# Second attention product of a windowed-attention kernel: 24 products on four 128x32 strips in place of 12 on two 128x64 tiles

## What is computed

```python
# batch 4, heads 8, seq 768, head_dim 64, chunk 32, left 16, right 8, 8 memory keys
for c in range(nc):                        # 24 chunks of 32 queries
    k_full = concat([mem_k, k_ctx])        # 8 + up to 56 = 64 keys
    v_full = concat([mem_v, v_ctx])
    scores = scale * q_c @ k_full.T
    a = softmax(scores)                    # 32 x 64
    out[:, :, c_start:c_end] = a @ v_full  # the second product, 32 x 64 x 64
x = attn_out as (3072, 512)
h = x @ w_in ; solu = h * softmax(h) ; ln = norm(solu) * g ; x2 = ln @ w_out
return leaky(x2 @ w_in2) @ w_out2
```

## Time and profile before

| | us |
|---|---|
| median of 3 runs | 803.44 |
| lowest, highest | 802.81, 803.88 |
| the profiled execution | 801.41 |
| its span, first to last instruction | 799.6 |
| TensorE busy | 792.2 |
| VectorE busy | 541.4 |
| ScalarE busy | 453.8 |

### The profile page before, as it was taken

How to read it: one execution, slowest core, us unless ns; L and a number is a source line. 1 busy time by engine, 2 the same in 40 slices (tenths; PEclk the granted TensorE clock), 3 DMA queues, 4 the chain that set the end, 5 groups by cost and what they waited for, 6 DMA issues and landing times.

```text
span 799.6 us, 14400 instructions
## 1 busy us (share of the span) xinstructions
PE 792.2 (99%) x5582; PEld 650.3 (81%) x5582; DVE 541.4 (68%) x902; ACT 453.8 (57%) x737; POOL 62.6 (8%) x156
## 2 busy tenths in 40 slices
PE   8999999999999999999999999999999999999998
PEld 5888888888888888888888888888888888888886
DVE  7988889987532656247452335666799698779775
ACT  4768887777443356255464447666645555545543
POOL 1233333322100000000000000000000000000000
PEclk9999999999999999999999999999999999999999
DMA  9956876865848875176774577545923740462002
GB/s 358 334 178 208 279 221 230 234 165 161 283 89 287 319 252 185 52 245 226 248 255 158 211 247 240 178 172 173 386 115 101 271 146 26 148 249 104 27 1 79
DMA packets 79892, 156.72 MB, mean 196 GB/s; under 512 B 6225, under 2 KB 30929, under 8 KB 79825
## 3 DMA queue, kind: packets, MB, share of 16 engines
q1 hardware_dynamic: 79824, 155.81, 57.7%
HBM read 99.16 MB, written 56.62 MB: 195 GB/s over the span
## 4 chain that ended last, share of the span: by engine, by line
PE 98%; DVE 1%; issue 0%; ACT 0%; POOL 0%; ACTq 0%
PE hid_a L732 24%; PE hid_b L732 24%; PE scores_ps L732 22%; PE attn_ps L732 14%; PE probs_ps L732 7%; PE attn_ps L724 3%; PE scores_ps L698 2%; PE probs_ps L710 1%; PE hid_b L846 0%; DVE unit_max L1164 0%; DVE shifted L1167 0%; DVE unit_sum L1176 0%; DVE w_in_lo L1146 0%; ACT prob L867 0%; POOL prob L1427 0%
## 5 line engine op out<-in xcount | busy, mean ns | idle before, releaser
L861 ACT ACTIVATE ring_hi<-g_blk 128x512 fp32r<-128x512 f32 x168 | 105.9, 632 | 108.1 <-PE hid_b L732 40.4
L1146 DVE TENSOR_TENSOR ring_lo<-g_blk,ring_hi 128x512 fp32r<-128x512 f32 x168 | 115.6, 688 | 38.6 <-ACT ring_hi L861 35.5
L1010 ACT ACTIVATE g_out<-g_out 128x512 f32<-128x512 f32 x72 | 45.4, 630 | 71.7 <-DVE g_out L1272 41.5
L732 PE MATMUL scores_ps<-x_op_P_hi,w_hi 128*128 128x512 f32 x144 | 56.1, 390 | 0.0
L732 PE MATMUL scores_ps<-x_op_P_lo,w_hi 128*128 128x512 f32 x144 | 56.0, 389 | 0.0
L732 PE MATMUL scores_ps<-x_op_P_hi,w_lo 128*128 128x512 f32 x144 | 56.0, 389 | 0.0
L732 PE MATMUL hid_b<-ring_hi,w_hi 128*128 128x512 f32 x128 | 49.9, 390 | 0.0
L732 PE MATMUL hid_b<-ring_lo,w_hi 128*128 128x512 f32 x128 | 49.8, 389 | 0.0
L732 PE MATMUL hid_b<-ring_hi,w_lo 128*128 128x512 f32 x128 | 49.8, 389 | 0.0
L1146 DVE TENSOR_TENSOR x_op_P_lo<-op_raw,x_op_P_hi 128x1024 fp32r<-128x1024 f32 x21 | 25.7, 1224 | 20.4 <-ACT x_op_P_hi L861 20.3
L732 PE MATMUL hid_a<-w_in_hi,xT_hi 128*128 128x512 f32 x96 | 39.4, 410 | 0.0
(11 more groups left out here) (178 smaller groups left out, 2041.0 us busy)
## 6 DMA issues: line engine op xcount, KB each, us to landing
g_scratch<-g_out SPq DMA_DIRECT2D x96, 256.0 KB, 2.6
g_blk<-g_scratch SPq DMA_DIRECT2D x48, 512.0 KB, 7.7
attn_buf<-qk_in SPq DMA_DIRECT2D x32, 576.0 KB, 6.6
attn_buf<-v_in SPq DMA_DIRECT2D x32, 384.0 KB, 4.3
ln_scratch<-lnT SPq DMA_DIRECT2D x24, 512.0 KB, 6.2
w_raw<-w_in SPq DMA_DIRECT2D x16, 512.0 KB, 4.1
ln_even<-ln_scratch SPq DMA_DIRECT2D x12, 512.0 KB, 6.7
ln_odd<-ln_scratch SPq DMA_DIRECT2D x12, 512.0 KB, 6.6
```

The costliest lines, as they stand in the source:

```text
L732: mm = pe.matmul(psum, weights[i], data[j], start=first and n == 0, stop=last and n == 2, skip_group_check=goes_on)
L861: return act.activation(dst, src, ACT.Copy)
L1010: act.activation(x, x, ACT.Prelu, alpha=0.01).then_inc(s_g[q], 1)
L1146: return ve.tensor_tensor(dst, x, hi.bitcast(f32), ALU.subtract)
```

## The change

The loop over the two heads becomes one over four strips. Each strip takes 32 of the 64 columns of the values as weights and writes 32 of the 64 partitions. Two strips share `n`, and so the same 64 moving columns. The products per unit go from 12 to 24, the columns streamed per tile remain the same, and so do all waits and the single count of `s_values` behind the last product.

```diff
--- before.py
+++ after.py
@@ -719,10 +719,10 @@
                 tokens = attn_ps[:, 0:BLOCK].rearrange("d (i a p q) -> d i p a q", i=3, a=2, p=2)
                 for i in range(3):
                     for p in range(2):
-                        for hb in range(2):
-                            n = 4 * i + 2 * p + hb
-                            mm = pe.matmul(tokens[64 * hb:64 * hb + 64, i, p],
-                                           buf[:, BLOCK + SEG + n * HEAD_DIM:BLOCK + SEG + (n + 1) * HEAD_DIM],
+                        for strip in range(4):
+                            n = 4 * i + 2 * p + strip // 2
+                            first = BLOCK + SEG + n * HEAD_DIM + strip % 2 * SQUARE
+                            mm = pe.matmul(tokens[SQUARE * strip:SQUARE * (strip + 1), i, p], buf[:, first:first + SQUARE],
                                            dg[:, n, :, :], start=True, stop=True)
                 mm.then_inc(s_values, 1)
```

## The result

The changed kernel takes 808.27 us (median of 4 runs, 806.14 to 808.77) against 803.63 for the kernel before; the ratio is 1.0054 with a 95% interval of 1.0038 to 1.007. The forecast was 802.3, and the range ended at 804.4. The stage itself became shorter, as forecast. What was lost lies in stops that the trace of the kernel before hardly has. The profiled executions lie further apart than the medians: 808.77 us is the longest of the four of the changed kernel, and 801.41 us is shorter than all four timed ones of the kernel before. The profiles thus account for 7.4 us, of which the medians show 4.6.

A forecast was written before the change was run, and what follows sets the result against it. TensorE was taken as the bound. Per unit -28 - 20 + 13 - 3 = -38 ns, times 30 units -1.15 us, from 803.44 to 802.3 us, "same"; range 801.3 to 804.4.

The forecast's parts named there:

- What bounds the kernel: Whole kernel: TensorE, busy 792.2 of 799.6 us; from 20 us on the stage's gains or losses reach the end one for one.
- Second round: Second round of passes in the attn_ps stage: starts 0.080 us behind the first instead of 0.108, -28 ns per unit.
- ten further rounds: Remaining rounds of the attn_ps stage: 56 ns each instead of 58, -20 ns per unit, bounded by -30 to 0.
- last round: End of the attn_ps stage: four strips start 7 ns apart in place of two, +13 ns per unit.
- rivals of serial tiles: attn_ps stage: loads not hidden, +6 us, 809.5, chance 4%; or only two full-height tiles at a time, +18 us, 822, 4%.
- vanished hand-over: Between attn_ps and scores: 0.13 of the 0.15 us goes, 3.4 us more gained, 798.9; chance 5%.
- the 0.15 us: From the last attn_ps pass's start to the first scores pass; cited as agreeing that a tiling mode change drains the engine.
- Times 30 units, -1.15 us: -38 ns per attn_ps stage over the 30 units that count, the first two being off the chain; ends -1.5 and -0.45 us.
- Twice as many instructions do the same work in the same number of rounds.: attn_ps stage: 24 products with 32 weight columns on four tiles replace 12 with 64 on two; 12 passes per tile remain.
- The supply rival: Scores behind attn_ps: too few passes stand ready, each missing one costs 17 ns, in 26 units; up to +7.8 us, 810; chance 16%.

## Why the prediction was wrong

1. *What bounds the kernel.* Right: PE bounds it, and a change on PE reaches the end one for one, in both directions.
2. *Second round, ten further rounds, last round.* Right. The row is 0.88 us long as forecast, so 0.70 became 0.66 us; four full-height strips run at once, and their loads lie under the passes. The rivals of serial tiles (4% each) and of the vanished hand-over (5%) are out: the hand-over is 0.80 - 0.66 = 0.14 us. One reading was too strong: the 0.15 us were taken as a drain of the array, but the first scores pass starts 0.07 us before the record of the last product ends (0.85 against 0.92 us in the earlier trace rows), and the ends of records are modelled, so a full drain is not shown.
3. *Times 30 units, -1.15 us.* Mis-sized. The period lost 16 ns and not 38, since the hidden products behind the scores take about 22 ns more. That makes about -0.5 us. Why they do is not shown.
4. *"Twice as many instructions do the same work in the same number of rounds."* This step failed. It gave 1,536 further instructions the price of nothing. In the profiled run 6.1 us of stops and 1.5 us of half clock stand against it. The denser stream made the block before 17.39 us last 3.9 us and not 6.1, and a block of the repeated part about 6.5 us and not 8.2. The runs with halved columns and with strips in three units alone show that more instructions at the start bring the long stop. Of its 4.59 us, 2.2 are PE's earlier arrival; the packet's later start is the rest, and its cause stays open. Nor does density explain the 1.13 us at 105.73, at the end of a block of 8.4 us.
5. *The supply rival (16%).* Right in name only: supply was the matter and the slower side came true. But it looked for it in the 17 ns per pass between two stages, with a price in each of 26 units. The scores kept their 0.50 us, so that mechanism did nothing. The real one works on 16 KB blocks, a few times in a run.
6. *What the profile before could have told.* The page had a queue called "instruction" with 44 packets, and its mean DMA share was 9 tenths in the first slices. The chain before had this inside a scores stage:

```profile
25.41 0.41 PE scores_ps L698 x33
25.81 0.05 issue
25.86 0.34 PE scores_ps L698 x15
```

   That is a stop of 0.05 us in mid-stage, two blocks on from 13.5 us. I read neither as a limit. The range (to 804.4) was set from terms of 0.5 to 3 us that all repeat by unit, and held no term for an event that happens once. It also took the spread of the kernel before from three executions (1.1 us), where later ones spread over 5 us.

What stays open: what sets the start of a block's packet among the other transfers (3.7 us after the last block's end in the kernel before, 5.9 in the changed one), since moving two loads did not move it; whether the dense stream itself delays it (it began 5.5 to 6.2 us after in four profiled programs with three dense stages at the start, but 3.4 in the one with padding ahead of them, and 5.5 in the run with every second unit, whose start is that of the kernel before); and why the same program meets it in one run and not in another.

## What to carry to other kernels

Count instructions as well as array time. An fp32 product is four of them, and cutting a stage into more products is free only while a block of 256 lasts clearly longer than its fetch, here 6 to 8.5 us under full DMA load. Look for the densest block and for the fullest transfers, which here met at the kernel's start. A stop in mid-stage with "issue" and no releaser is the sign. What bears it out is the same count of passes and loads in two kernels, and a packet on the instruction queue that ends a little before PE goes on.

## What the runs showed of the hardware

- TensorE stopped at the ends of blocks of 256 instructions, in seven of the programs after the same 347 or so passes and as many loads. In all 21 such stops of 0.1 us or more behind 9 us, in nine programs, it went on 1.2 to 1.6 us after the end of a packet on the instruction queue. The longest stop was 4.84 us.
- 16 KB of instructions took 0.9 to 2.2 us on the queue once begun. In the changed kernel they began 5.9 us after the block before was used up, with the transfers at over 400 GB/s, and with the loads held back (249 and 261 GB/s from 12 to 14 us) 2.3 and 1.3 us after.
- 128x32 tiles of full height run four at a time, with a record of 64 fp32 columns on each in about 56 ns a round (48 records in 0.66 us), as 64x32 tiles do in eights.
- 1,648 semaphore increments on TensorE's queue (48 in each of 32 units, 112 at the start) cost 104 us, about 63 ns each, and so are no neutral padding.
